# Query copies, key products and weight splits moved in the order of ScalarE, VectorE and GpSimd in a fused attention and MLP kernel

## The reference

```python
for t in range(S):                                  # B, H, S, D = 4, 8, 768, 48
    cur = np.einsum('bhd,bhe->bhde', u[None] * kt, vt)
    y[:, :, t] = np.einsum('bhd,bhde->bhe', rt, state + cur)
    state = wt[:, :, :, None] * state + np.einsum('bhd,bhe->bhde', kt, vt)
x = y as (3072 tokens, 384)
x = silu(norm(x) @ w_gate) * (norm(x) @ w_val) @ w_out     # d_ff 1536, the gated MLP
x = (s * relu(x @ w_in) ** 2 + b) @ w_out2                 # d_ff 2048, the squared MLP
```

## Time and profile before

| | us |
|---|---|
| median of 3 runs (lowest, highest) | 1008.15 (1006.68, 1008.67) |
| the profiled execution | 1008.67 |
| its span | 1006.9 |
| PE busy | 983.7 (98%) |
| DVE busy | 558.8 (55%) |
| ACT busy | 331.5 (33%) |
| POOL busy | 273.5 (27%) |

### The profile page before, as it was taken

One profiled execution on the slowest core, in us unless ns is written; L12 is line 12 of the kernel. 1 busy time (PEld: TensorE's weight loads), 2 busy tenths in 40 slices (PEclk: granted clock), 3 DMA queues, 4 the chain that ended last, 5 costly groups with the idle time before them and its releaser, 6 DMA issues.

```text
span 1006.9 us, 23059 instructions
## 1 busy us (share of the span) xinstructions
PE 983.7 (98%) x9704; PEld 820.2 (81%) x9704; DVE 558.8 (55%) x783; ACT 331.5 (33%) x570; POOL 273.5 (27%) x199
## 2 busy tenths in 40 slices
PE   7887999999999999999999999999999999999998
PEld 7775888888888888888888888888888888888898
DVE  6788876874876587558753225506337054162440
ACT  1452323232423333242323445405225043161340
POOL 4653733462545265334610560000000000000000
PEclk7799999999999999999999999999999999999999
DMA  7380244025211601450116201011020110201000
GB/s 279 114 328 4 75 140 134 2 91 161 98 49 61 208 33 49 128 172 3 49 52 216 88 23 63 1 26 38 11 52 0 21 42 10 52 0 21 12 8 24
DMA packets 70778, 73.97 MB, mean 73 GB/s; under 512 B 50464, under 2 KB 55072, under 8 KB 69408
## 3 DMA queue, kind: packets, MB, share of 16 engines
q1 hardware_dynamic: 70112, 71.52, 22.6%
q10 hardware_dynamic: 576, 1.14, 0.3%
HBM read 59.27 MB, written 13.37 MB: 72 GB/s over the span
## 4 chain that ended last, share of the span: by engine, by line
PE 86%; DVE 0%; issue 0%; ACT 0%; DVEq 0%
PE value_o_ps L676 13%; PE mix_gate_ps L676 13%; PE o_ps L1592 11%; PE level_ps L47 10%; PE o_ps L688 9%; PE mix_gate_ps L1592 5%; PE mix_gate_ps L47 5%; PE value_o_ps L47 5%; PE value_o_ps L688 4%; PE level_ps L524 2%; PE o_ps L1605 2%; PE mix_gate_ps L624 2%; PE level_ps L624 2%; PE level_ps L511 1%; PE mix_gate_ps L1605 1%; PE value_o_ps L1605 1%
## 5 line engine op out<-in xcount | busy, mean ns | idle before, releaser
L1368 POOL TENSOR_TENSOR R<-R,arena 128x512 f32<-128x512 f32 x72 | 113.5, 1587 | 183.0 <-PE level_ps L511 74.8
L1691 DVE SCALAR_TENSOR_TENSOR sqr<-relu,sb_col 128x512 f32<-128x512 f32 x96 | 72.3, 753 | 73.2 <-ACT relu L1653 73.2
L1215 DVE TENSOR_TENSOR u_raw<-value_o_ps,u_raw 128x512 f32<-128x512 f32 x66 | 45.4, 688 | 103.4 <-PE value_o_ps L676 103.4
L909 ACT ACTIVATE u_hi<-u_raw 128x512 fp32r<-128x512 f32 x66 | 41.7, 632 | 173.3 <-DVE u_raw L1215 173.3
L902 ACT ACTIVATE u_raw<-mix_gate_ps 128x512 f32<-128x512 f32 x72 | 43.0, 598 | 148.7 <-PE mix_gate_ps L676 148.6
L676 PE MATMUL mix_gate_ps<-x_hi,w_hi 128*128 128x512 f32 x216 | 85.5, 396 | 1.0 <-DVE w_lo L1200 0.9
L676 PE MATMUL value_o_ps<-x_hi,w_hi 128*128 128x512 f32 x216 | 85.6, 397 | 0.0
L676 PE MATMUL mix_gate_ps<-x_lo,w_hi 128*128 128x512 f32 x216 | 84.2, 390 | 0.0
L676 PE MATMUL value_o_ps<-x_hi,w_lo 128*128 128x512 f32 x216 | 84.2, 390 | 0.0
L676 PE MATMUL mix_gate_ps<-x_hi,w_lo 128*128 128x512 f32 x216 | 84.2, 390 | 0.0
L676 PE MATMUL value_o_ps<-x_lo,w_hi 128*128 128x512 f32 x216 | 84.1, 390 | 0.0
(11 more groups left out here) (221 smaller groups left out, 2360.9 us busy)
## 6 DMA issues: line engine op xcount, KB each, us to landing
kr_nat<-kr SPq DMA_DIRECT2D x10, 1152.0 KB, 5.8
K<-kT SPq DMA_DIRECT2D x12, 512.0 KB, 4.5
arena<-wT SPq DMA_DIRECT2D x12, 512.0 KB, 6.3
R<-rT SPq DMA_DIRECT2D x10, 512.0 KB, 3.9
w_raw<-wgv SPq DMA_DIRECT2D x12, 384.0 KB, 5.5
v_sb<-v SPq DMA_DIRECT2D x12, 384.0 KB, 4.3
x_scratch<-x_sb SPq DMA_DIRECT2D x18, 256.0 KB, 2.3
x_raw<-x_scratch SPq DMA_DIRECT2D x6, 768.0 KB, 4.3
```

What stands on the lines that cost most here:

```text
L1215: dve.tensor_tensor(u[:, f % 2], value_ps[:], u[:, f % 2], ALU.mult).then_inc(u_done, 1)
L1368: pool.tensor_tensor(q, q, decay(blk, l, 0), ALU.mult).then_inc(rmul_done, 1)
L1691: dve.scalar_tensor_tensor(out=sq[f % 2][:], in0=relu[f % 2][:], scalar=sb_col[:, 0:1], in1=relu[f % 2][:], op0=ALU.mult, op1=ALU.mult).th ...
```

## The change

ACT does the weight roundings of block 1 ahead of the query copies of the same step. In every block from 1 on, `upper_queries(s, 0)` and `fourth_queries(s, 1)` go from step 5 to step 6, and `upper_queries(s, 1)` from step 6 to step 8. On DVE `place_lower` goes behind `multiply_keys` and `advance_first` of the same step; in block 1 the decays of level 2 are made at step 2 in place of step 3, `lower_weights(2)` is made at step 3 in place of step 2, the other late splits go to the end of their steps, and one of them from step 25 to step 21. On POOL `own_next` goes from between the two level-2 products of the queries (step 6) to the end of step 3. PE's and SP's instructions keep their order.

```diff
-LATE_OUT = (8, 13, 16, 25, 27)
+LATE_OUT = (8, 13, 16, 21, 27)
...
         def attention(s, k):          # ScalarE
+            if s == 1 and k in (1, 3, 5, 7):
+                upper_weights(8 + k // 2)
+            if s == 1 and k in (2, 4, 6, 8):
+                upper_out_weights(1 + k // 2)
             if k == 0:
                 odd_queries(s, 1)
...
             if k == 4:
                 fourth_queries(s, 0)
-            if k == 5:
+            if k == 6:
                 upper_queries(s, 0)
                 fourth_queries(s, 1)
-            if k == 6:
+            if k == 8:
                 upper_queries(s, 1)
-            if s == 1 and k in (1, 3, 5, 7):
-                upper_weights(8 + k // 2)
-            if s == 1 and k in (2, 4, 6, 8):
-                upper_out_weights(1 + k // 2)
...
                 lower_out_weights(0)  # VectorE
-            if k == 1 and s > 1:
+            if k == (2 if s == 1 else 1):
                 decays_after(s, 1)
-            if k == 2 and s == 1:
+            if k == 3 and s == 1:
                 lower_weights(2)
             if k in LOWER_AT:
                 blk = LOWER_AT.index(k)
-                place_lower(s, blk)
-                if s == 1 and blk == 0:
-                    decays_after(s, 1)
                 multiply_keys(s, 1, blk)
                 advance_first(s, blk)
+                place_lower(s, blk)
...
-            if s == 1 and k in LATE_WEIGHTS:
-                lower_weights(3 + LATE_WEIGHTS.index(k))
-            if s == 1 and k in LATE_OUT:
-                lower_out_weights(1 + LATE_OUT.index(k))
...
                 attention_out(s, 3)
+            if s == 1 and k in LATE_WEIGHTS:
+                lower_weights(3 + LATE_WEIGHTS.index(k))
+            if s == 1 and k in LATE_OUT:
+                lower_out_weights(1 + LATE_OUT.index(k))
...
-                multiply_queries(s, l, [0])   # GpSimd
-                if l == 2:
-                    own_next(2 * s)
-                multiply_queries(s, l, [1])
+                multiply_queries(s, l)
                 if l == 1:
                     carry_queries(s, 0)
                     carry_queries(s, 1)
+                    own_next(2 * s)
```

## The result

The changed kernel takes 1014.25 us (median of 4 runs, 1013.17 to 1015.19) against 1007.70 of the kernel before in the runs beside it. The ratio is 1.0064, with a 95% interval of 1.0047 to 1.0083: about 6.5 us slower. The forecast was 1014.8.

What follows compares the result with a forecast made beforehand. PE, busy 98% of the span, was taken to bound the kernel. Blocks 2 to 5 add 5.0 us, block 1 0.5, step 24 0.9: 6.4 us, forecast 1014.8 us, likeliest range 1011.8 to 1017.

Steps and rivals of the forecast that it cites:

- likeliest case: Whole kernel: slower, 1014.8 us forecast, within 1011.8 to 1017; chance 0.66.
- The chain in blocks 2 to 5: Before `middle_levels(0)`: PE waits for the query copy behind ACT's rounding, 1.25 us a block, 5.0 in all.
- Port: DVE's key products in blocks 2 to 5 run undisturbed, 0.7 us each, since POOL stands still behind its first level-2 product.
- `own_next` on `u_lo` of tile 0: Blocks 2 to 5, step 3: may set `u_lo` back by at most 1.84 us; counted free, but close.
- Block 1, steps 2 to 10: Some waits swallowed, others new, at the weight splits and `middle_levels(0)`: +0.5 us, bounds -1.0 and +2.0.
- the fourth wait: Block 1, output product of tile 2: PE comes at 92.2 and waits for its weight split, taken to end at 93.2.
- The clock: Block 1: the stretch at 1.2 of 2.4 GHz behind the waits, costing 1.7 us, stays in.
- Step 24: Block 1: the split moved to step 21 delays the states `attend(0)` waits for: +0.9 us, between 0.7 and 1.1.
- The sum: 5.0 + 0.5 + 0.9 = 6.4 us slower, bounds 3.7 and 9.5.
- The gain of block 1 wins: Rival: DVE freed of POOL removes block 1's four waits and half-clock stretch, -7.8; net -1.9, 1006.5 us; chance 0.09.

Runs made afterwards that it cites:

- e2: Kernel before with only ACT's query copies moved, from steps 5 and 6 to steps 6 and 8; 1014.88 us, ratio 1.0063.
- e1: Changed kernel with ACT's query copies back at their old steps 5 and 6; 1008.32 us, ratio to before 1.0008.
- e10: Changed kernel with ACT's step 6 turned round, the query copies issued ahead of the rounding of `u`; 1005.04 us, ratio to before 0.9968.
- e7: Kernel before with only POOL's `own_next` moved to the end of step 3; 1007.96 us, ratio 1.0001.
- e3: Changed kernel with the split of output weights at step 25 again in place of 21; 1013.09 us, ratio to before 1.0055.
- e5: Kernel before with `own_next` and `own_keys` of block 1 behind the level-3 query products, and splits at steps 7 and 8 swapped; 1004.54 us, ratio 0.9966.
- e11: e10 with the output-weight split back at step 25, and `own_next` and `own_keys` of block 1 at level 3; 1004.22 us, ratio to before 0.9960.
- e4: Changed kernel with POOL's `own_next` back between the level-2 products of the queries; 1014.25 us, ratio to before 1.0063.
- e6: Kernel before with only POOL's `own_next` and `own_keys` of block 1 moved behind the level-3 query products; 1007.65 us, ratio 0.9999.
- e9: e5 with the weight split of tile 3 in block 1 ahead of the key products of half 1; 1005.01 us, ratio to before 0.9970.
- e8: Kernel before with DVE's key products ahead of masked copies, and block 1's decays at step 2, tile 2 split at 3; 1006.61 us, ratio 0.9989.

## Why the prediction was right

Its likeliest case came true, at the place and by the mechanism it named.

- **The chain in blocks 2 to 5.** Forecast: 1.25 us a block, 5.0 in all. Measured: four waits, 4.7 us together, and 1.25, 1.09, 1.26 and 1.22 us more for the blocks (the last to the end of the kernel), 4.8 in all. Its pieces, from the rows of the changed kernel: DVE starts 1.33 us behind `lower_levels(1)`, key products 1.07, masked copies 2.18, to the rounding 0.76, to the copy 0.54. e2 shows that this one edit does it, e1 that undoing it takes it away, and e10 that it is the place behind the rounding that counts.
- **Port.** DVE's key products ran undisturbed, since POOL stood still, as argued. But `own_next` and the order on DVE have no part in it: in e2 both are as before, and the key product of half 1 still took 0.68 us, and PE waited 1.33 us. It is the late query copy itself that holds POOL back, and the move of `own_next` ahead was not needed for it.
- **`own_next` on `u_lo` of tile 0.** Called free but close, and it is: in blocks 2 to 5 `u_lo` is blocked for 1.6 us, and PE doesn't wait (e7). In block 1 of e10 PE waited 2.13 us for it.
- **Block 1, steps 2 to 10.** Forecast +0.5 us (bounds -1.0 and +2.0). Measured: steps 0 to 18 are 1.1 us shorter, just outside, and 1.5 in the trace of e3. The pieces up to `middle_levels(0)` hold, with waits of 1.54, 0.83 and 2.73 where the shift was put at 2.0, 3.0 and 2.0 (it is 1.5, 2.5 and 1.5 in the traces, set against the first L524 of each). The term that is off is the last one, the wait of 1.0 us for the split before the output product of tile 2. I put the split's end at 93.2, and it ended at 90.6 (91.6 on the forecast's scale, since this trace starts block 1 1.0 us earlier), 1.6 us ahead of PE. DVE and POOL there:

```profile
68.72 2.40 DVE L1026 TENSOR_TENSOR arena<-arena 128x256 f32<-128x256 f32 x2
...
89.64 0.94 DVE L1205 TENSOR_TENSOR wo_lo<-wo_raw,wo_hi 128x768 fp32r<-128x768 f32 x1
```

```profile
68.21 2.29 POOL L1377 TENSOR_TENSOR kr_nat<-kr_nat 128x768 f32<-128x768 f32 x1
...
91.01 1.10 POOL L1366 TENSOR_TENSOR R<-R,arena 128x512 f32<-128x512 f32 x1 [2.38 <-ACT x_raw L848]
92.07 1.85 POOL L1391 TENSOR_TENSOR kr_nat<-kr_nat 128x768 f32<-128x768 f32 x1
```

The first row is `own_next` holding the decays, as forecast (2.40 us for 0.74). But `own_products` runs at 92.07, behind the split, where before it ran in front: the level-3 product at 91.01 waits for `upper_queries(1)`, which the change moved to step 8, and `own_products` is queued behind it. I counted POOL's work as late and in the way, and here it was so late as to be out of it.

This is not the order alone; the clock has a part in it. PE ran at its lower clock behind the wait of 2.73, and the gate activation of tile 3, and `upper_queries(1)` behind that, came late with it: 6.10 us behind `middle_levels(0)`. In e3, the same program up to there with the same three waits (1.55, 0.83 and 2.77), the granted clock stayed full and that copy came 4.71 us behind. PE, DVE and POOL of e3:

```profile
84.86 1.15 PE L524 MATMUL level_ps<-y,K 64*64 64x48 f32 x64 [2.77 <-ACT y L848]
...
92.44 0.47 PE L688 MATMUL o_ps<-u_hi,wo_hi 128*128 128x512 f32 x1 [0.95 <-DVE wo_lo L1205]
```

```profile
90.42 1.88 DVE L1205 TENSOR_TENSOR wo_lo<-wo_raw,wo_hi 128x768 fp32r<-128x768 f32 x1
```

```profile
90.36 1.12 POOL L1366 TENSOR_TENSOR R<-R,arena 128x512 f32<-128x512 f32 x1 [0.95 <-ACT x_raw L848]
91.44 2.56 POOL L1391 TENSOR_TENSOR kr_nat<-kr_nat 128x768 f32<-128x768 f32 x1
```

There POOL's level-3 product falls on the split, which takes 1.88 us for 0.94, and PE waits 0.95 us, the fourth wait as forecast. So the forecast of this wait holds where the clock stays full. What the sum had wrong is to count the wait and a fall of the clock one on top of the other: a fall ahead of the output product takes the place of the wait.

- **The clock.** A stretch at the lower level was left in, and one is there, from 85.8 to 89.2 us, behind the wait of 2.73; two of its rows are

```profile
86.00:87.00 1.00, 1.00 (x3) 0.50 0.00 0
...
89.00:90.00 1.00, 1.00 (x5) 0.90 0.00 0
```

where it was at 93 to 97 before. At half speed PE loses about 1.7 us in it, as it did before. But it isn't fixed by the order: e3 has no such stretch, and its steps 0 to 18 are only 0.4 us shorter, since the fourth wait stands there instead.

- **Step 24.** Forecast +0.9, measured 1.08 against 0.23 us of waiting, and 0.84 by e3.
- **The sum.** By the two traces: -0.3 for block 1 with step 24 (-1.1 + 0.8), +4.8 for blocks 2 to 5, and -1.0 for block 0, which the change doesn't touch and which differs from execution to execution: together 3.5, as between the spans. Forecast was +6.4. The timed runs give 6.5, with an interval of 4.7 to 8.3. That the total fits better than block 1 does is luck; the forecast's own sum with block 1 corrected is 4.7, at the low end of the interval. From the first gated matmul of block 1 to the end the two traces differ by 4.5 us, 2.0 less than the medians of the timed runs. In eleven of the twelve changed kernels this distance, set against the trace of before, gives 0.3 to 2.0 us less than the medians do; e10 is the exception. That points to a stretch in the one trace of before that was slower than usual, rather than to a further cost of the change, but nothing shows it. It stays open.
- **The rivals.** "The gain of block 1 wins" was wrong here, but its mechanism is real: e5 and e11 take 3.4 and 4.1 us off the kernel before by moving POOL's work in block 1. Its price of 7.8 us was about twice what was got in time; in the trace of e11 steps 0 to 18 are 6.9 us shorter, and 1.4 us of that are given back behind them.

## What to carry to other kernels

- A copy that PE waits for must not stand in an in-order queue behind an instruction that waits for another engine, however short that one is. The idle time that ACT showed in front of its rounding, 5.6 us, was the warning, and the two timelines gave the price to a tenth of a microsecond.
- In a stretch where PE has no idle time, a move can only be free or cost; in a stretch with several waits in a row, taking one away mostly makes the next one longer (e4, e6, e7, e9). The gains of 3 us and more came from several edits together (e5, e9, e10, e11).
- When an instruction is made later on purpose, follow the queue behind it as well: what it releases comes late too, and that can help. It isn't a safe gain: of two traces of the same stretch one had the wait for the split (e3) and one had not.

## What the runs showed of the hardware

- The time until the first gated matmul of block 1 is the same program in all thirteen kernels, and it lay between 58.8 and 61.9 us in their traces. A single trace can't carry a verdict of less than some 3 us here. Distances within a trace are better: block 2, where its order was as before, took 93.56 to 93.70 us (before, e5, e6, e9). In block 1 even they differ for the same program, 55.76 against 55.35 us for steps 0 to 18.
- DVE and POOL block each other for whole instructions: in block 2 of the changed kernel `u_lo` took 2.33 us for 0.69 while `own_next` ran, ending 0.55 us behind it, and `own_next` took 2.02 us for 1.84. In blocks 2 to 5 of the changed kernel this never reached PE.
- PE's granted clock fell to its lower level at or behind single waits of 2.1 us (e10), 2.3 (e1), 2.7 (the changed kernel), 2.8 (e7), 3.3 (e6), 3.6 (e4) and 4.1 (e2). It did not fall behind one of 2.77 in e3, at the same place and behind the same waits as that of the changed kernel, so the length of the wait doesn't settle it. In the kernel before it fell behind a wait of 1.7 us, the last of four in block 1 (at 79.4, 83.6, 85.6 and 92.8). It stayed full through block 1 in e5, e8, e9 and e11, whose longest wait there was 1.7 us, and behind the four waits of 1.17 us in blocks 2 to 5.
- How long it stayed low did not follow the wait either: it cost 1.7 us of full speed behind 2.1, 2.3, 2.7 and 3.6 us, and stayed low for some 7 us, twice as long, at 2.8, 3.3 and 4.1.
